# An MLP's first product by seven block products instead of eight, with the low halves of its gates on GpSimd

## What is computed

```
def _moe_ref(x, domain_probs, w1, w2):        # w1 (4, 512, 1024), w2 (4, 1024, 512)
    p = domain_probs / (domain_probs.sum(-1, keepdims=True) + 1e-09)
    out = np.zeros((N, D), dtype=np.float32)
    for e in range(E):
        h = np.maximum(x @ w1[e], 0.0)
        out += p[:, e:e + 1] * (h @ w2[e])
    return out

def _moe2_ref(x, w_in, w_out):                # w_in (512, 2048), w_out (2048, 512)
    h = x @ w_in
    g = h * np.cos(h)
    return g @ w_out
```

## Time and profile before

| | us |
|---|---|
| median of three runs | 811.57 |
| the profiled execution | 811.25 |
| its span | 809.5 |
| TensorE busy | 802.3 |
| VectorE busy | 581.0 |
| ScalarE busy | 291.9 |
| GpSimd busy | 227.9 |
| DMA busy, mean in the MLP | about a tenth |

### The profile page before, as it was taken

The page is one execution under the profiler, slowest core; times in us unless marked ns, Lnnn a source line. Parts: engine busy times, 40 slices in busy tenths (PEclk is TensorE's granted clock), DMA queues, the critical chain, the costliest instruction groups (busy, mean ns, idle before and its releaser), DMA issues.

```text
span 809.5 us, 11379 instructions
## 1 busy us (share of the span) xinstructions
PE 802.3 (99%) x4404; PEld 677.6 (84%) x4404; DVE 581.0 (72%) x962; ACT 291.9 (36%) x548; POOL 227.9 (28%) x230
## 2 busy tenths in 40 slices
PE   8999999999999999999999999999999999999998
PEld 7888888888888888888888888888888888888886
DVE  6887766766766767767667658577777787777766
ACT  4743222222222222322222322246454554545442
POOL 3976343334333333433433433242000000000000
PEclk9999999999999999999999999999999999999999
DMA  8941100120110111101011011000011001100004
GB/s 326 334 151 56 50 27 27 40 78 27 40 38 27 40 66 40 40 27 40 28 39 40 27 39 40 27 27 28 26 40 40 27 27 40 39 27 28 1 0 156
DMA packets 19865, 44.83 MB, mean 55 GB/s; under 512 B 2344, under 2 KB 2392, under 8 KB 19812
## 3 DMA queue, kind: packets, MB, share of 16 engines
q1 hardware_dynamic: 19812, 44.10, 16.6%
HBM read 40.93 MB, written 3.17 MB: 54 GB/s over the span
## 4 chain that ended last, share of the span: by engine, by line
PE 97%; DMA 1%; POOL 1%; DVE 1%; SPq 0%; ACT 0%; issue 0%
PE ps L1020 33%; PE ps L1001 28%; PE ps L1082 16%; PE ps L1101 16%; PE ps L968 1%; PE ps L918 1%; DMA att<-att_in 1%; PE ps L932 1%; PE ps L955 1%; POOL h_lo L440 1%; PE ps L942 1%; DVE att L661 0%; SPq L288 0%; DVE temps L795 0%; DVE y L865 0%; DVE temps L753 0%
## 5 line engine op out<-in xcount | busy, mean ns | idle before, releaser
L440 POOL TENSOR_TENSOR h_lo<-temps,h_hi 128x512 fp32r<-128x512 f32 (+1 forms) x128 | 135.3, 1058 | 295.3 <-ACT h_hi L540 295.2
L540 ACT ACTIVATE h_hi<-temps 128x512 fp32r<-128x512 f32 (+1 forms) x128 | 67.3, 526 | 336.9 <-DVE temps L758 336.9
L741 DVE TENSOR_TENSOR y<-ps,y 128x512 f32<-128x512 f32 x180 | 124.0, 689 | 71.8 <-PE ps L1020 71.8
L1020 PE MATMUL ps<-h_hi,w_hi 128*128 128x512 f32 x384 | 150.5, 392 | 0.1
L1001 PE MATMUL ps<-x_hi,w_hi 128*128 128x512 f32 (+1 forms) x448 | 150.4, 336 | 0.1
L1001 PE MATMUL ps<-x_hi,w_lo 128*128 128x512 f32 (+1 forms) x448 | 150.5, 336 | 0.0
L1001 PE MATMUL ps<-x_lo,w_hi 128*128 128x512 f32 (+1 forms) x448 | 150.5, 336 | 0.0
L1020 PE MATMUL ps<-h_lo,w_hi 128*128 128x512 f32 x384 | 150.3, 391 | 0.0
L1020 PE MATMUL ps<-h_hi,w_lo 128*128 128x512 f32 x384 | 149.4, 389 | 0.0
L1001 PEld LDWEIGHTS ps<-x_hi,w_hi 128*128 128x128 f32 x448 | 84.7, 189 | 12.8 <-DVE temps L772 0.3
L1001 PEld LDWEIGHTS ps<-x_lo,w_hi 128*128 128x128 f32 x448 | 84.7, 189 | 11.7
(11 more groups left out here) (84 smaller groups left out, 1113.3 us busy)
## 6 DMA issues: line engine op xcount, KB each, us to landing
w_raw<-w_in SPq DMA_DIRECT2D x96, 256.0 KB, 2.6
att<-att_in SPq DMA_DIRECT2D x24, 512.0 KB, 7.0
temps<-p_scr SPq DMA_DIRECT2D x4, 768.0 KB, 4.0
out<-y SPq DMA_DIRECT2D x12, 256.0 KB, 2.0
att<-dp_in SPq DMA_DIRECT2D x1, 24.0 KB
p_scr<-att SPq DMA_DIRECT2D x1, 24.0 KB
lam<-lam_in SPq DMA_DIRECT2D x1, 6.0 KB, 1.6
```

What stands on the lines that cost most here:

```text
L440: pool.tensor_tensor(hs_lo[side][:, f, at], ring(s, i), f32(hs_hi[side][:, f, at]), ALU.subtract).then_inc(s_hlo, 1)
L540: act.activation(hs_hi[s % SIDES][:, f, at], ring(s, i), ACT.Copy).then_inc(s_hhi, 1)
L741: dve.tensor_tensor(at, from_bank, at, ALU.add).then_inc(s_y, 1)
L1020: mm = pe.matmul(ps[:, DOWN_BANK + g % DOWN_BANKS, :], ww[:, s // SIDES % 2, f, at], hh[side][:, f, tokens], start=(f == 0 and n == 0), st ...
```

## The change

The MLP gets the experts' scheme. Its quarters become steps 32 to 47, again with a side of 512 and one of 256 columns and seven products each, in the order P1, P5, P6, P2, P7, P4, P3.

- **Bank 1 opens with P1.** ScalarE copies P1 from bank 0 into bank 1, and P6 accumulates on top of it; u2 and u3 are then plain copies of the bank by ScalarE.
- **Gate from SBUF.** c11 and c21 are copied by ScalarE into the ring in SBUF, c12 and c22 are sums of VectorE into the ring. The turns, both subtractions and the gate read the ring instead of a bank.
- **Lows of the gates** are made by GpSimd's `h_low`, as the experts' are; the MLP's weights get their four sums on GpSimd too.
- **The T sums of the MLP's x** (four per side) are made at the border by VectorE, with highs on ScalarE and lows on VectorE and GpSimd. The table FOLLOW_LAST brings the evictions of step 31 forward.
- **Downs** follow products by the function `follow`: in step 32 four downs behind P5, in step 33 none, in step 34 eight, and from then on four in a side 0 step and eight in a side 1 step; eight are left for the end.

```diff
+MLP_STEP = (P1, P5, P6, P2, P7, P4, P3)
+FOLLOW_LAST = ((), (), (0, 1), (2, 3), (4, 5, 6, 7), (), ())
...
+def follow(s):
+    if s == STEPS:
+        return (), ((s - 1, 0), (s - 1, 1), (s - 1, 2), (s - 1, 3)), (), (), (), (), ()
+    if s == STEPS + 1:
+        return (), (), (), (), (), (), ()
...
+    if s > STEPS and s % SIDES == 0:
+        return ((s - 2, 4),), (), ((s - 2, 5),), ((s - 2, 6),), ((s - 2, 7),), (), ()
+    if s > STEPS:
+        return (((s - 2, 0),), ((s - 2, 1),), ((s - 2, 2),), ((s - 2, 3),), ((s - 1, 0),), ((s - 1, 1),),
+                ((s - 1, 2), (s - 1, 3)))
...
+            def before_p6(s):
+                act.wait_ge(s_prod, product_count(s, P1))
...
+                    act.wait_ge(s_c21, s - STEPS)
+                act.activation(ps[:, 1, 0:CTS[s % SIDES]], ps[:, 0, 0:CTS[s % SIDES]], ACT.Copy).then_inc(s_pre, 1)
...
             def product(s, i):
 
                 w, x, bank, opens = PRODUCTS[i]
+                if i == P6 and s >= STEPS:
+                    opens = False
...
+                    if i == P5:
+                        if s == STEPS:
+                            pe.wait_ge(s_t, 3 * s)
+                        else:
+                            pe.wait_ge(s_c, 2 * (s - STEPS))
...
+                    if i == P6:
+                        pe.wait_ge(s_pre, s - STEPS + 1)
+                        if s == STEPS:
+                            pe.wait_ge(s_x2lo, 8)
...
+                    if i == P7:
+                        pe.wait_ge(s_u2, s - STEPS + 1)
...
+                    if i == P4:
+                        pe.wait_ge(s_u3, s - STEPS + 1)
...
+                    if i == P3:
+                        pe.wait_ge(s_c, 2 * (s - STEPS) + 1)
```

More of the change, by code:

```diff
@@ new lines, in _ @@
+            for s in range(STEPS, ALL_STEPS):
+                q, side = s // SIDES, s % SIDES
+                more = q + 1 < ALL_QUARTERS
+                before_p6(s)
+                if s == STEPS:
+                    x2_high(0, 4)
+                    x2_t_high(0, 1)
+                    x2_t_high(0, 2)
+                    x2_t_high(0, 3)
+                    for d in range(KT):
+                        x2_high(1, d)
+                sine(s - 1, 3)
+                take_u2(s)
+                if s == STEPS:
+                    x2_high(1, 4)
+                    x2_t_high(1, 0)
+                gate_high(s - 1, 2)
+                if more and side == 0:
+                    w1_piece(q + 1, 0)
+                elif more:
+                    w1_piece(q + 1, 2)
+                take_c11(s)
+                turns(s, 0)
+                take_u3(s)
+                if s == STEPS:
+                    x2_t_high(1, 1)
+                    x2_t_high(1, 2)
+                    x2_t_high(1, 3)
+                gate_high(s - 1, 3)
+                turns(s, 1)
+                sine(s, 0)
+                take_c21(s)
+                turns(s, 2)
+                if more and side == 0:
+                    w1_piece(q + 1, 1)
+                elif more:
+                    w2_piece(q + 1, 0)
+                gate_high(s, 0)
+                sine(s, 1)
+                turns(s, 3)
+                sine(s, 2)
+                if more and side == 1:
+                    w2_piece(q + 1, 1)
+                gate_high(s, 1)
@@ L783, in _ @@
                     down(s - 1, 0)
+                if last:
+                    down(s - 1, 1)
                 if s:
@@ L789, in _ @@
                     weighted(s, 0, bank_a)
-                if side == 1:
+                if last:
+                    down(s - 1, 2)
+                    down(s - 1, 3)
+                elif side == 1:
                     down(s - 1, 1)
@@ L800, in _ @@
                     weighted(s, 0, bank_a)
-                if side == 1:
+                if last:
+                    down(s - 1, 4)
+                elif side == 1:
                     down(s - 1, 2)
@@ L817, in _ @@
                 sum_of(s, 2, bank_b, p1)
-                if side == 1:
+                if side == 0:
+                    down(s - 1, 2)
+                elif not last:
                     down(s - 1, 4)
-                else:
-                    down(s - 1, 2)
                 dve.wait_ge(s_t, 3 * s + 2)
@@ L825, in _ @@
                     w1_piece(1, 2)
-                elif side == 0 and 0 < q < QUARTERS - 1:
+                elif side == 0 and q:
                     w1_piece(q + 1, 2)
-                if side == 1:
+                if side == 1 and not last:
                     down(s - 1, 5)
@@ L831, in _ @@
                 sum_of(s, 3, bank_c, v2)
-                if side == 1:
+                if side == 0:
+                    down(s - 1, 3)
+                elif not last:
                     down(s - 1, 6)
-                else:
-                    down(s - 1, 3)
                 if s != 0:
@@ new lines, in gate, with evict @@
+            def gate(s, i):
+                m = 4 * (s - STEPS) + i
+                if m < 0:
+                    return
+                dve.wait_ge(s_sq, m + 1)
+                dve.scalar_tensor_tensor(out=ring(s, i), in0=rr[:, m % K_RING, 0:CTS[s % SIDES]], scalar=1.0,
+                                         in1=ring(s, i), op0=ALU.subtract, op1=ALU.mult).then_inc(s_gate, 1)
+            def evict(s, k):
+                held = [t for place in follow(s) for t in place]
+                if k < len(held):
+                    down(*held[k])
@@ L907, in _ @@
+            less_turns(ALL_STEPS - 1, 3)
+            down(ALL_STEPS - SIDES, 4)
+            gate(ALL_STEPS - 1, 2)
+            gate(ALL_STEPS - 1, 3)
+            for i in range(5, 8):
+                down(ALL_STEPS - SIDES, i)
+            for i in range(4):
+                down(ALL_STEPS - 1, i)
         @block.tensor
@@ L1116 @@
+            for i in range(4, 8):
+                down(ALL_STEPS - SIDES, i)
+            for i in range(4):
+                down(ALL_STEPS - 1, i)
 def kernel(q, k, v, lam, moe_domain_probs, moe_w1, moe_w2, moe2_w_in, moe2_w_out):
```

467 lines of the change are left out of this document (274 added, 193 removed).

## The result

The changed kernel takes 849.47 us (848.8 to 850.63, four runs) against 811.5 of the kernel before on the same chip: a ratio of 1.047, 95% interval 1.045 to 1.049. The forecast of 836 had the sign right; the time lies 1.5 us beyond the upper end of its range. The profiled run took 849.18 us, with a span of 847.3.

What follows compares the result with a forecast made beforehand. TensorE was taken as the bound. In turns, -13.1 + 21.9 + 5 x 3.95 + 1.3 = +29.9 (841.1 us); without, +9.7 (820.9); three quarters of the difference gave 836, range 814 to 848.

Steps and rivals of the forecast that it cites:

- The view of the bound and the prices: Whole kernel: TensorE bounds nearly throughout; VectorE and ScalarE instruction times by width, such as 0.68 us on VectorE at 512 columns.
- the 13.1 us for the columns: MLP: fewer up-matmul columns save 1.66 us in each of 8 quarters, less 0.2 for an extra matmul.
- The steady quarter in turns: Steady MLP quarters: VectorE and GpSimd alternate on SBUF reads, c22 comes late, P5 waits 3.1 us; quarter 34.9 us.
- Without turns: Steady MLP quarter if VectorE and GpSimd don't hold each other: P5 waits 1.1 us, quarter 32.7 us.
- the walk: MLP border and steady quarter: instructions laid out by hand in queue order at the priced times, giving each wait.
- The border in turns: MLP's first steps, 32 to 35: TensorE waits for T sums, lows and copies, 21.9 us with VectorE and GpSimd alternating.
- The figure without turns at the border, 13.5: Steps 32 to 35: TensorE's waits if VectorE and GpSimd don't alternate, 3.1, 9.6 and 0.8 us.
- three quarters of the difference: Whole kernel: 836 us chosen between 820.9 without turns and 841.1 with all turns, expecting some collisions to fall away.
- the third rival: MLP border: TensorE's clock falls to half for some 8 us of matmuls, adding 4 us; 840 to 845, chance 0.12.
- Rare turns: MLP: VectorE and GpSimd seldom hold each other; 821 us (815 to 826), chance 0.18.
- keeping up: MLP: the other engines keep out of TensorE's way, c22 ready in time; 801 us (797 to 808), chance 0.09.
- the most likely case: MLP: most of the turns between VectorE and GpSimd are taken; 827 to 845 us, chance 0.55.

Runs made afterwards that it cites:

- b3: Changed kernel with c22's sum and P1's copy moved earlier, and GpSimd's MLP gate lows and weight sums done for one column only: 818.11 us.
- a1: Changed kernel plus thrown-away matmuls before P5 in step 33 (24) and side 1 steps from 37 on (12), keeping TensorE's clock up: 846.08 us.
- a2: Changed kernel with GpSimd's MLP gate lows, and weight sums from the MLP's second quarter on, done for one column only: 828.38 us.
- c1: Changed kernel plus 24 thrown-away matmuls before step 33's P5 only, none in the steady quarters: 848.08 us.
- d1: b3 with GpSimd's x lows at the MLP's border also replaced by writing zeros: 813.26 us.
- b1: Changed kernel with GpSimd's four weight sums per MLP quarter moved from before side 0's c22 into side 1's step, same work: 840.69 us.
- b2: b1 plus c22's sum moved earlier on VectorE and P1's copy earlier on ScalarE: 830.96 us, run again 830.10 us.

## Why the prediction was wrong

**The view of the bound and the prices** held. So did the 13.1 us for the columns: b3's quarters are 31.02 against 30.98, and the border and the columns add up to its time.

**The steady quarter in turns** held nearly instruction by instruction. From P1 the walk has c22 at 20.17, the trace at 20.25 (675.92 - 655.67). P5's wait is 3.1 in the walk, which counts from a matmul's turn, and 3.08 in the trace, which counts from the end of its record, 0.16 later: 3.2 by the walk's measure. At full clock (a1) the quarter is 35.3 against 34.9. Without turns, 32.7 against 32.75 in a2, P5's wait 1.1 against 0.93 + 0.16.

**The border in turns** held as far as it goes:

| | walk | trace |
|---|---|---|
| step 32: P1, downs, P6 | 1.2, 0.65, 3.0 | 1.31, 0.22, 2.73 |
| step 32: P4, P3 | 1.9, 2.5 | 1.01, 1.85 |
| step 32 ends | 564.2 | 564.27 |
| step 33: P5, with c22 at | 5.9, 570.8 | 5.74, 570.8 |
| step 33: P6, P4, P3 | 1.9, 1.75, 1.5 | 0.98, 0.47, 0.64 |
| step 34 starts | 580.3 | 581.14 |
| third MLP quarter starts | 617.7 | 619.77 |

The waits of the trace are again 0.16 short by the walk's measure. P4 and P3 of step 32 and P6, P4 and P3 of step 33 wait less than that, since TensorE itself is at half rate there: the clock's time and the waits' time overlap. At the full level (c1) they are 1.52, 2.31, 1.66, 1.48 and 1.25, near the walk's 1.9, 2.5, 1.9, 1.75 and 1.5. The figure without turns at the border, 13.5, assumed GpSimd's x lows out of the way too. a2 and b3 leave them in, and have some 21 and 18.8; d1 has 14.3.

**The step that failed** is the one behind the working: "Turn-taking was seen, but the phases are mine, and some collisions fall away where GpSimd comes early or late. I take three quarters of the difference". No collision fell away: P5 waited 3.06 to 3.08 us in each of the five steady quarters, so the phase of one quarter was that of the next. The walk's own sum in turns, 841.1, stood in the text, and I cut 5 us off it for a reason without a row. That is 5.1 of the 13.5 us by which 836 missed.

**The second step that failed** is the third rival, by place and by size. "TensorE's clock falls at the border", 4 us there, chance 0.12. It did fall, at the border (0.72 in the window from 564 us on) and in every steady quarter behind a P5 wait of 3.1 us, which the walk itself had set out and to which I gave no clock price. By size: step 33's matmuls ran at half rate from 570.9 to 579.2 us, the 8 us that the rival had, but that cost 0.7 us (c1); in five quarters 5 x (36.04 - 35.27) = 3.8 us (a1). I had taken the matmuls' lost time as loss, but part of it only fills a wait that would have followed. The Trainium skill ("TensorE: Matmul & The Clock Gate", section "HAM oscillation — how this bites in real kernels") has long gaps bring half rate back; the trace agrees, at 0.21 instead of 0.12 us per matmul of 256 columns after a gap of 3.08 us, but not every time: in c1 one gap of 3.08 us was followed by the full level. What it would cost had to be taken from a1.

**The rest**: 849.18 less 841.1 is 8.1, of which the clock has 3.8 + 0.7 = 4.5. The other 3.6 or so lie in three places: in a1, at full clock, the steady quarters are still 0.35 longer than the walk's (5 x 0.35 = 1.7), the border without the clock's 0.7 has some 1.4 us more than the walk, and the last quarter lost some 2 us where the walk has 1.3. Why, stays open.

**The other rivals.** Rare turns (821) and keeping up (801) are out: P5 waited over 3 us for c22 in every steady quarter, and where the shown one has holds of 0.3 to 1.1 us, a2 has none. "VectorE becomes the bound: 849" named the measured time, but not its cause. VectorE isn't full: b1 and b2 leave its instructions as they are, move its work and GpSimd's, and lose 9 and 19 us.

**The range** was too narrow at the top for a reason that can be seen in the text: the most likely case had two additions left out (full turns +5, clock in the quarters +4) and both push the same way.

## What to carry to other kernels

Fewer columns on TensorE are worth nothing if a bank's reader comes late: before a scheme is moved to another stage, walk the queue of the engine that frees the bank, and put the sums and copies that free banks ahead of work that nobody waits for. If a periodic loop's walk gives a number, take all of it, not a share, and add what each wait in it does to the clock. A stage that has to prepare operands at its start (here 14.3 to 24.0 us of border) must save more than that in its steady part; 8 quarters x 1.66 us were too few.

Whether the new scheme can win with a first MLP quarter by the old scheme, which would hide the T sums, was not tried. By an estimate it would be level at best: b2's border costs 22.1 us (its third quarter starts at 617.91, where TensorE's work alone would put it at 595.8), so with nothing lost there it would take about 808, and a first quarter of the old kind gives 1.7 of that back.
